# Channel mix of a fused attention, experts and channel mix kernel: the second product with seven half-size products (Strassen) in place of eight

## What is computed

```python
def _moe2_ref(x, mu_k, mu_r, w_k, w_v, w_r):            # x: 4 x 544 x 512
    x_prev = np.concatenate([np.zeros((B, 1, D)), x[:, :-1, :]], axis=1)
    xk = mu_k * x + (1.0 - mu_k) * x_prev
    xr = mu_r * x + (1.0 - mu_r) * x_prev
    k = np.maximum(xk @ w_k, 0.0)                        # 512 -> 1024
    v = k * k @ w_v                                      # 1024 -> 512, the second product
    r = 1.0 / (1.0 + np.exp(-(xr @ w_r)))                # 512 -> 512, the gate
    return r * v
```

## Time and profile before

| | |
|---|---|
| median of 3 runs | 613.18 us (611.17 to 622.49) |
| the profiled execution | 616.3 us, span 614.4 us |
| granted clock of TensorE, mean | 0.983 |
| PE busy | 567.6 us, 92% |
| PE weight loads busy | 470.5 us, 77% |
| DVE busy | 308.8 us, 50% |
| ACT busy | 300.4 us, 49% |
| POOL busy | 147.0 us, 24% |
| channel mix | from 372 us to the end |

### The profile page before, as it was taken

How to read it: one execution, slowest core, us unless ns; L and a number is a source line. 1 busy time by engine, 2 the same in 40 slices (tenths; PEclk the granted TensorE clock), 3 DMA queues, 4 the chain that set the end, 5 groups by cost and what they waited for, 6 DMA issues and landing times. The chain is left out here.

```text
span 614.4 us, 15300 instructions
## 1 busy us (share of the span) xinstructions
PE 567.6 (92%) x6100; PEld 470.5 (77%) x6100; DVE 308.8 (50%) x764; ACT 300.4 (49%) x799; POOL 147.0 (24%) x240
## 2 busy tenths in 40 slices
PE   3989988788988999999999889899999999999997
PEld 2667666566855987797697688798898989898996
DVE  3667776594355345445527735562635435261511
ACT  1678777695455345435535538262524334251501
POOL 4644445551375112213323223000000000000000
PEclk9989999899996999999999999999999999999999
DMA  9985989850321000000000004000000000000000
GB/s 187 214 168 79 238 140 227 131 93 2 87 70 36 2 1 2 1 0 0 1 18 1 2 2 138 28 7 35 1 35 1 36 17 18 18 18 34 2 35 17
DMA packets 68991, 32.89 MB, mean 54 GB/s; under 512 B 55744, under 2 KB 63936, under 8 KB 68928
## 3 DMA queue, kind: packets, MB, share of 16 engines
q1 hardware_dynamic: 68928, 32.00, 24.4%
HBM read 27.54 MB, written 4.46 MB: 52 GB/s over the span
## 5 line engine op out<-in xcount | busy, mean ns | idle before, releaser
L44 PE MATMUL ps_H<-XH,w_kL 128*128 128x256 f32 (+1 forms) x288 | 81.1, 282 | 1.0 <-ACT square L1571 1.0
L45 PE MATMUL ps_H<-XL,w_kH 128*128 128x256 f32 (+1 forms) x288 | 80.8, 280 | 0.0
L46 PE MATMUL ps_H<-XH,w_kH 128*128 128x256 f32 (+1 forms) x288 | 80.8, 280 | 0.0
L1571 ACT ACTIVATE square<-ps_H 128x512 f32<-128x512 f32 (+1 forms) x36 | 20.6, 573 | 120.8 <-PE ps_H L46 107.3
L44 PEld LDWEIGHTS ps_H<-XH,w_kL 128*128 128x128 f32 x288 | 54.3, 189 | 1.8 <-ACT square L1571 1.2
L44 PE MATMUL ps_V<-w_vH,HL 128*128 128x512 f32 x136 | 53.1, 390 | 1.8 <-DVE HL L1625 1.8
L45 PEld LDWEIGHTS ps_H<-XL,w_kH 128*128 128x128 f32 x288 | 54.3, 189 | 0.3
L46 PEld LDWEIGHTS ps_H<-XH,w_kH 128*128 128x128 f32 x288 | 54.3, 189 | 0.0
L45 PE MATMUL ps_V<-w_vL,HH 128*128 128x512 f32 x136 | 53.0, 390 | 0.0
L46 PE MATMUL ps_V<-w_vH,HH 128*128 128x512 f32 x136 | 52.9, 389 | 0.0
L1120 ACT ACTIVATE probs_m<-ps_H,nmax_m 128x128 f32<-128x128 f32 (+3 forms) x64 | 33.2, 523 | 31.7 <-DVE nmax_m L1274 31.6
(11 more groups left out here) (245 smaller groups left out, 1487.6 us busy)
## 6 DMA issues: line engine op xcount, KB each, us to landing
VW<-in_v_l_dram SPq DMA_DIRECT2D x32, 336.0 KB, 6.6
out_dram<-gate SPq DMA_DIRECT2D x17, 256.0 KB, 2.0
QKraw<-in_k_l_dram SPq DMA_DIRECT2D x16, 256.0 KB, 5.3
QKraw<-in_q_l_dram SPq DMA_DIRECT2D x16, 256.0 KB, 5.3
raw_b<-in_moe_w_k_dram SPq DMA_DIRECT2D x8, 256.0 KB, 2.6
raw_c<-in_moe_w_v_dram SPq DMA_DIRECT2D x6, 256.0 KB, 2.8
raw_b<-in_moe_w_r_dram SPq DMA_DIRECT2D x4, 256.0 KB, 2.8
raw_qkv<-in_moe_wq_dram SPq DMA_DIRECT2D x1, 512.0 KB, 7.3
```

The lines of the kernel that those rows point to most:

```text
L44: nc.tensor.matmul(out, al, bh, start=(starts and k == 0), stop=False)
L45: nc.tensor.matmul(out, ah, bl, start=False, stop=False)
L46: last = nc.tensor.matmul(out, ah, bh, start=False, stop=(ends and k == n - 1))
L1571: nc.scalar.activation(square[:, g % 2, 0:2 * n], ps_H[:, g % 2, 0:2 * n], ACT.Relu).then_inc(relued, 1)
```

## The change

The second product is done by halves of the tokens (t), of the features (k) and of the outputs, in Winograd's form of Strassen's identity: seven products of 128 tokens by 512 features by 256 outputs. Four of the seven weight blocks and four of the seven activation blocks are sums, made in fp32 before they are split into rounded half and rest. So `hidden` pairs feature block g with g + 4; `work` holds nine blocks of 128 columns per group, of which seven are split; `mixed` has one buffer, used for xk and then for xr, and lends its space to w_v's loads. GpSimd makes the sums of w_v, in one buffer of four (`sums`), which the chunks use later for partial results. The products share three banks of PSUM: ScalarE copies a bank out before the next product is added on it (`see`), VectorE combines the copies (`results`). The last chunk, of 128 tokens, does five plain products.

```diff
 def hidden(nc, keep, g, k, n):
-    f = slice(P * (2 * g + k), P * (2 * g + k) + P)
+    f = slice(P * (g + 4 * k), P * (g + 4 * k) + P)
...
+        NB, HF = 7, FC // 2
+        B11, B21, B22, T1, T2, T3, T4 = range(NB)
+        A22, A11, A12, S1, S2, S4, S3 = range(NB)
+        WVH, WVL = m.sbuf("w_vH", [P, NB, HF, 256], FP32R), m.sbuf("w_vL", [P, NB, HF, 256], FP32R)
+        HH, HL = m.sbuf("HH", [P, NB, HF, P], FP32R), m.sbuf("HL", [P, NB, HF, P], FP32R)
+        sums = m.sbuf("sums", [P, 4, 256])
+        mixed = m.sbuf("mixed", [P, DC, CH])
+        work = m.sbuf("work", [P, 2, 9, P])
+        ps_V = m.psum("ps_V", [P, 3, 512])
+        place = [gate[:, :, :], mixed[:, :, :].rearrange("p (a b) n -> p a (b n)", a=2)]
...
             @block.sync
+                rows = w_v.rearrange("(k j p) n -> j p k n", k=2, p=P)
+                for j in range(HF):
+                    if j >= 2:
+                        sp.wait_ge(w_lo, j - 1)
+                        sp.wait_ge(t_made, j - 1)
+                    sp.dma_start(place[j % 2], rows[j]).then_inc(raw_loaded[j % 2], 16)
...
             @block.tensor
+                def product(bank, a, w, starts, ends):
+                    n = HF
+                    for j in range(n):
+                        for k, (x, y) in enumerate(((HL, WVH), (HH, WVL), (HH, WVH))):
+                            last = nc.tensor.matmul(ps_V[:, bank, 0:256], x[:, a, j, :], y[:, w, j, :],
+                                                    start=(starts and j == 0 and k == 0),
+                                                    stop=(ends and j == n - 1 and k == 2), skip_group_check=True)
+                    return last
...
                     pe.wait_ge(h_lo, 4 * c + 4)
+                    if c == 0:
+                        pe.wait_ge(w_lo, HF)
+                        pe.wait_ge(wt_lo, HF)
+                    else:
+                        pe.wait_ge(mixed_out, 3 * c)
+                    if n < CH:
+                        product(0, A22, B11, True, False)
+                        product(0, A11, B21, False, True).then_inc(v_done, 1)
+                        product(1, A22, B11, True, False)
+                        product(1, A22, T1, False, False)
+                        product(1, A11, B22, False, True).then_inc(v_done, 1)
+                        return
+                    v, k = 7 * c, 4 * c
+                    product(0, A11, B11, True, False).then_inc(v_done, 1)
+                    product(1, A12, B21, True, True).then_inc(v_done, 1)
+                    pe.wait_ge(seen, k + 1)
+                    product(0, S2, T2, False, False).then_inc(v_done, 1)
+                    product(2, S1, T1, True, False).then_inc(v_done, 1)
+                    pe.wait_ge(seen, k + 2)
+                    product(0, S3, T3, False, False).then_inc(v_done, 1)
+                    pe.wait_ge(seen, k + 3)
+                    product(2, S4, B22, False, True).then_inc(v_done, 1)
+                    pe.wait_ge(seen, k + 4)
+                    product(0, A22, T4, False, True).then_inc(v_done, 1)
...
             @block.scalar
                 def shift(c, which):
-                    if c > 1:
-                        act.wait_ge((xk_lo, xr_lo)[which], c - 1)
+                    if which:
+                        act.wait_ge(xk_lo, c)
+                    elif c > 1:
+                        act.wait_ge(xr_lo, c - 1)
...
+                def weight_hi(j):
+                    act.wait_ge(raw_loaded[j % 2], 16 * (j // 2 + 1))
+                    src = place[j % 2]
+                    nc.scalar.activation(WVH[:, B11, j, :], src[:, 0, 0:256], ACT.Copy)
+                    nc.scalar.activation(WVH[:, B21:B22 + 1, j, :], src[:, 1, :].rearrange("p (k n) -> p k n", k=2),
+                                         ACT.Copy).then_inc(w_hi, 1)
+
+                def sum_hi(j):
+                    act.wait_ge(t_made, j + 1)
+                    nc.scalar.activation(WVH[:, T1:T4 + 1, j, :], sums[:, :, :], ACT.Copy).then_inc(wt_hi, 1)
+
+                def see(c):
+                    for k, (done, bank) in enumerate(((1, 0), (3, 0), (4, 2), (5, 0))):
+                        act.wait_ge(v_done, 7 * c + done)
+                        if k == 0:
+                            if c == 0:
+                                act.wait_ge(wt_lo, HF)
+                            else:
+                                act.wait_ge(mixed_out, 3 * c)
+                        nc.scalar.activation(sums[:, (0, 1, 3, 2)[k], :], ps_V[:, bank, 0:256], ACT.Copy).then_inc(seen, 1)
...
                 def chunk(c):
                     for g in range(FC // 2):
+                        if later(c) and g == 1 and c:
+                            shift(c + 1, 0)
+                        relu(c, g)
                         if g:
+                            hidden_hi(c, g - 1)
+                        if c == 0:
+                            weight_hi(g)
+                            sum_hi(g)
+                    hidden_hi(c, FC // 2 - 1)
+                    if c == 0:
+                        act.wait_ge(w_lo, HF)
+                        act.wait_ge(t_made, HF)
+                        shift(1, 0)
                     if later(c):
                         split_k(c + 1)
...
                     if later(c):
+                        shift(c + 1, 1)
                         split_r(c + 1)
+                    if n == CH:
+                        see(c)
...
             @block.gpsimd
+                for j in range(HF):
+                    src = place[j % 2]
+                    b11, b12, b21, b22 = src[:, 0, 0:256], src[:, 0, 256:512], src[:, 1, 0:256], src[:, 1, 256:512]
+                    pool.wait_ge(raw_loaded[j % 2], 16 * (j // 2 + 1))
+                    if j:
+                        pool.wait_ge(wt_lo, j)
+                    nc.gpsimd.tensor_tensor(sums[:, 0, :], b12, b11, ALU.subtract).then_inc(t_step, 1)
+                    nc.gpsimd.tensor_tensor(sums[:, 2, :], b22, b12, ALU.subtract)
+                    pool.wait_ge(t_step, 2 * j + 1)
+                    nc.gpsimd.tensor_tensor(sums[:, 1, :], b22, sums[:, 0, :], ALU.subtract).then_inc(t_step, 1)
+                    pool.wait_ge(t_step, 2 * j + 2)
+                    nc.gpsimd.tensor_tensor(sums[:, 3, :], b21, sums[:, 1, :], ALU.subtract).then_inc(t_made, 1)
...
             @block.vector
+                def square(c, g):
+                    n, m4 = size(c), 4 * c + g + 1
+                    dve.wait_ge(relued, m4)
+                    w = work[:, g % 2, :, :]
+                    if n < CH:
+                        nc.vector.tensor_tensor(w[:, 1:3, :], w[:, 1:3, :], w[:, 1:3, :], ALU.mult).then_inc(summed, 1)
+                        return
+                    nc.vector.tensor_tensor(w[:, 0:4, :], w[:, 0:4, :], w[:, 0:4, :], ALU.mult).then_inc(squared, 1)
+                    dve.wait_ge(squared, m4)
+                    nc.vector.tensor_tensor(w[:, 7:9, :], w[:, 2:4, :], w[:, 0:2, :], ALU.subtract).then_inc(differed, 1)
+                    nc.vector.tensor_tensor(w[:, 4, :], w[:, 0, :], w[:, 1, :], ALU.add)
+                    dve.wait_ge(differed, m4)
+                    nc.vector.tensor_tensor(w[:, 5, :], w[:, 1, :], w[:, 7, :], ALU.subtract)
+                    nc.vector.tensor_tensor(w[:, 6, :], w[:, 8, :], w[:, 7, :], ALU.add).then_inc(summed, 1)
...
                 def chunk(c):
                     for g in range(FC // 2):
+                        if c == 0:
+                            weight_lo(g)
+                        square(c, g)
                         if g:
+                            hidden_lo(c, g - 1)
+                        if c == 0:
+                            sum_lo(g)
+                        if later(c) and g == 2 and c:
+                            mix(c + 1, 0, mixed_k)
+                    hidden_lo(c, FC // 2 - 1)
+                    if c == 0:
+                        mix(1, 0, mixed_k)
                     if later(c):
                         split_lo(c + 1, 0)
+                        mix(c + 1, 1, mixed_r)
                         split_lo(c + 1, 1)
+                    results(c)
```

160 lines of the change are left out of this document (67 added, 93 removed).

## The result

| | before | after |
|---|---|---|
| median | 615.12 us (6 runs) | 674.49 us (6 runs, 669.95 to 683.33) |
| ratio | | 1.096, 95% interval 1.091 to 1.102 |
| the profiled execution, its span | 616.3, 614.4 us | 669.95, 668.1 us |
| granted clock, mean | 0.983 | 0.964 |
| PE busy | 567.6 us, 92% | 574.7 us, 86% |

The change costs 59 us.

The account below looks back on a forecast made before the run. TensorE was taken to bound the kernel. First chunk 23.0 + 1.7, chunks 1 to 6 21.3 + 0.6, chunk 7 1.0, last chunk 1.7, clock 5: +54 us, 670 profiled or 667 against the median; range 644 to 684.

Parts of the forecast that it names:

- What bounds the kernel: Channel mix before the change: TensorE busy 28.00 of 28.00 us, VectorE 12.39, ScalarE 10.90.
- What it takes away: TensorE's second product: 9.97 us a full chunk, 0.93 less, 7.5 over 8 chunks; last chunk +1.67.
- The steady chunk: Chunks 1 to 6: stalls of 1.2 us before the first product, 3.25 before the third; period 31.4, +3.55 each.
- The floor: Steady chunks: chain from ps_R's end through sigmoid, shift, mix, split_r, copy, 5.7 us; at least +1.95 per chunk, 11.7 in all.
- The first chunk: Weight loading and sums in four rounds of about 6.5 us; first product at 403.0, +23.0 us before the clock's part.
- The clock: TensorE's clock falls after stalls, 1.7 us each: +1.7 in the first chunk, 5 in chunks 1 to 6.
- The last chunk: 128 tokens: five products take 7.12 us in place of 5.45, +1.67 us.
- TensorE decides everything: Rival: first copy and sums come in time, only -5.8 us remains, 607 us; chance 0.03.
- Only the first chunk pays: Rival: copies in time in steady chunks, round of sums stands, +20 us, 633; chance 0.07.
- The floor (648): Rival: floor of the chain, rounds of 5.5 us, no clock fall in steady chunks, +35 us, 648; chance 0.2.
- clock at every second stall and rounds of 7.5 us: Rival: clock falls at every second stall, first-chunk rounds take 7.5 us, +63 us, 676; chance 0.2.
- My own walk: The prediction's own case, instruction queues walked in order: 655 to 672 us; chance 0.5.

Follow-up runs that it names:

- e13: Three edits of order, a first chunk of plain products, and relu in its own buffer, on the changed kernel: 627.19 us, 1.023 of the kernel before.
- filled gap: Changed kernel plus 22 unread TensorE instructions between second product and wait for the first copy, chunks 1 to 6: 666.12 us, 1.089 of the kernel before.
- narrow-product run: Kernel before, second product of full chunks as seven narrow products, one of eight quarters left out, no sums or copies: 607.77 us, ratio 0.987.
- three edits of order: Changed kernel with copies ahead of split_r, xk mixed one group earlier, next chunk's first hidden group between products two and three: 638.56 us, ratio 1.037.
- e3: Changed kernel with VectorE mixing the next chunk's xk one group earlier, ahead of square 1: 674.28 us, 1.096 of the kernel before.
- e5: Changed kernel without GpSimd's weight sums, blocks filled from the loaded weights instead: 663.67 us, 1.079 of the kernel before.
- e12: e5 with GpSimd's 16 sums back in a buffer nobody reads; only the next load and first shift wait for them: 669.53 us, ratio 1.090.

## Why the prediction was right, point by point

**The sum.** The forecast was +54 us; measured are 59.4 by the medians and 60.9 in the phase. The kinds of loss and their places were right, and the miss of 6.6 us has three parts: 2.7 in the first chunk, 3.8 in chunks 1 to 7, most of it the clock, and 0.1 in the last chunk.

**What bounds the kernel.** Right: TensorE, with two engines half idle. The run with all orders put right and relu's own buffer (e13) shows the steady chunk bound by TensorE once more, at 27.04 us.

**What it takes away.** Right in kind, a little too large: 10.05 to 10.07 us for seven products against my 9.97 (0.83 us saved, not 0.93). The pace of ps_H carried over to within 1%.

**The steady chunk.** Right at both places. The first stall in the changed kernel is 1.2 to 1.35 us (walked: 1.2), the second 3.0 to 3.1 (3.25), the period without a fall of the clock 31.4 to 31.7 (31.4 and the memset). Over chunks 1 to 6 that is +22.4 us against my +21.9, chunk 7 +1.15 against +1.0. Prices by interpolation held: hidden_hi 0.95 us, hidden_lo 1.08, a copy 0.37, a shift 1.70. The new square ran 1.76 us (455.65 to 457.41) against 1.74. One sentence of it was a wrong reading: that VectorE works "without a break" from square 2 to hidden_lo 3 was true as a timeline, but I took it as the cause of the first stall. Earlier mixing won 0.36 us; the cause is the loop relu, square, HL, relu through two buffers, 3.48 us a turn, which I had walked through (relu(2) waits for HL) without naming it.

**The floor.** I took the chain behind the gate, 5.7 us, as what no speed of VectorE in the hidden layer shortens. No run tests that: in the changed kernel the chain's shift waited for VectorE's XL (468.43 above) and not for the gate. And it is a floor only for that order of the queues. Moving two copies took 30 us away.

**The first chunk.** +27.4 us against +24.7; beside the clock this is the term that missed most. The first product came 33.0 us behind the first relu (walked: 30.9): 0.8 us in the first round, from the load of 512 KB, which landed 4.1 us behind that relu and not 3.2, and 1.3 us from the three later rounds (7.1 to 7.3, walked 6.5 to 7.0). The hold-up of VectorE beside GpSimd was named and priced at 0.4 to 0.7 us for two or three instructions a round; the comparison with the run without sums puts it at 5.4 us for the four rounds. The wait of ps_H for the relu of group 1, 5.4 us, was not walked; nothing hangs on it. The low clock behind the second idle time cost 2.5 us (9.67 us for five products of 7.2), I had 1.7.

**The clock.** Right that it falls at some of the second stalls, four of six in the profiled execution (I took half), too small in size: 1.5 us twice and 2.6 twice, 8 us in all, where I had 5. The filled gap confirms 8. My price per fall, 1.7 us, came from one row; here the low clock lasted 3.4 us or 6.9, and cost 1.5 or 2.6.

**The last chunk.** +1.74, as worked out (+1.67).

**Rivals.** TensorE decides everything (607): the narrow-product run shows what it would have given, 607.8, so that the number was right and its condition, copies and sums in time, was not. Only the first chunk pays (633): this asks for steady chunks 0.93 us shorter than before; the nearest is e13, 627.2, with chunks 0.81 us shorter and a cheaper first chunk, while the three edits of order only bring the period back to the 27.8 of the kernel before. The floor (648): rounds took 7.2 us and not 5.5, and the clock fell. The last, clock at every second stall and rounds of 7.5 us (676), came nearest: 674.5 measured, four falls of six and rounds of 7.1 to 7.3. My own walk, 655 to 672, was given 0.5 and lies just below the result.

**What stays open.** Why the low clock lasts 3.4 us in some chunks and 6.9 in others of the same execution; in chunk 2 it began 1.4 us behind the start of the third product, in chunk 5 0.9 us ahead of it. And why with the same idle time it falls in some chunks and not in others. And whether any order of the first chunk would let the seven products win: they save 0.8 us a chunk, and in the best run the first chunk, even done plainly, costs 18 us more than in the kernel before (42.15 us from the phase's first ps_H of TensorE, 374.69, to that of chunk 1, 416.84, where 24.4 stood). That run is still 2.3% slower than the kernel before. Sums made in an earlier phase, where GpSimd and VectorE have time, weren't tried.

## What to carry to other kernels

An eighth fewer products is not an eighth less time: here it was 8% of the second product and 3% of a chunk, since instructions of half the columns took more than half the time (120 ns where 512 columns took 227), and it has to be paid for by additions on other engines. Before counting these as hidden because an engine is half idle, walk its queue in order: a copy that stands behind another engine's answer stalls TensorE by the whole chain, and moving it ahead of one instruction was worth half the loss. And price one-time preparation by itself; here it takes 18 us in the best run, more than all the chunks together can give back (6.6).

## What the runs showed of the hardware

- VectorE and GpSimd hold each other up in the instructions seen here, which on both engines take two inputs from SBUF: 512 columns on VectorE 0.68 us alone and 1.22 beside GpSimd, 1024 columns 1.22 and up to 1.78; 256 columns on GpSimd 0.73 alone and 1.05 to 1.7 beside VectorE. It happens for results that nobody reads, too. The Trainium skill (GPSIMD Engine Reference, Specifications) names the cause, an SBUF interface shared with VectorE for instructions with two SBUF inputs; that VectorE's stretch is 5.5 us longer with unread sums than without agrees with it.
- TensorE's clock fell to 1.2 GHz at idle times of 2.8 to 3.1 us in four of six chunks, stayed up in the other two with the same idle time, and came back after 3.4 or 6.9 us. In the profiled executions of e3, e5 and e12, with the same idle time in each chunk, it fell in six, four and three of six. In the steady chunks it never fell at 1.0 to 1.4 us.
- In a stream with new weights each time, 256 columns take 119 to 120 ns, 128 columns 111 and 512 columns 227: from 256 to 128 columns there is next to nothing to win.
